# Windowed attention and two MLPs on one core: the order of query tiles, the position of the value products and the step where the MLP begins

## The chip, the cores and the metric

The kernel runs on one core of a Trainium2 chip. The metric is the device time of one execution in microseconds (us); less is better. TensorE is written PE in the rows, VectorE DVE, ScalarE ACT, GpSimd POOL, and SyncE, which issues most of the DMAs, SP.

## The reference

```python
B, H, Sl, D = 4, 8, 512, 64;  Sg = 32;  window = 32
# attention: 32 global and 512 local positions of each of 32 heads
s_g  = scale * q_g @ concat(k_g, k_l).T            # global queries see all 544 keys
out_g = softmax(s_g) @ concat(v_g, v_l)
s_ll = where(|i - j| <= window, scale * q_l @ k_l.T, -1e9)
s_lg = scale * q_l @ k_g.T                         # local queries see the 32 global keys
out_l = softmax(concat(s_lg, s_ll)) @ concat(v_g, v_l)
x = concat(out_g, out_l) as [B, 544, 512]
# first MLP, 512 -> 2048 -> 512, with layer norm and residual
x = x + relu(((x - mu) / sqrt(var + 1e-6) * g_ln) @ w_ch1) @ w_ch2
# second MLP, 512 -> 1024 -> 512, with a 3-tap convolution over positions as a gate
h = relu(x @ w_in);  out = (h * sigmoid(conv3(h))) @ w_out
```

All inputs and the output are float32.

## The kernel before, in words

Every engine's program is one loop over the same steps `s` (0 to END-1). Each step has slots for several pieces of work, and semaphores order the engines; no scheduler moves anything, so the order written in the loop is the order on the engine.

**Attention** takes steps 0 to 66. Step s treats two heads (a pair p of heads, kept together in `two[...]` and `vv[...]`) and one tile t of 128 local queries. On TensorE a step holds `scores(s)` (2 matmuls with 64 rows of contraction; they stand in the trace as tiles 64\*128), `transposes(s-2)` (4 transposes of the exponentials, 128\*128) and `values(s-3)` (16 small matmuls into 32-partition pieces of the output bank, 128\*32). Between them DVE takes the masked row maximum (`row_max`, L736), ACT the exponentials (`exponents`, L926 and L929) and the copy of the transposed exponentials out of PSUM (`probabilities`, L952). After each second step DVE divides by the row sums (`read_out`, L768 to L776) into `x_loc`. For each group G of four heads there are also the global queries: `global_scores` (8 matmuls, called a burst here), `global_max`, `global_exponents`, two extra transposes (G0, G1) and `global_values`. From G = 2 on the scores of the burst's step come late in it, behind the MLP's up-projection.

**The MLP** has 104 units: `up(n)` (12 matmuls of 256 or 384 columns, from the layer-normed x and the hi and lo parts of the weights) and `down(n)` (6 or more matmuls of 512 columns). Unit n stands in step `U0 + n`, and `down` one step later. With U0 = 23, steps 23 to 66 hold attention and MLP together. PSUM is short: before U0 attention alternates between two banks for transposes and for outputs, and the same banks are `u_ps` for the MLP from U0 on, after which each has one bank. Row statistics (`half_sums`, `variances` on DVE, `inverse_deviation` on POOL), `ln_rows` on DVE, and the transposes called LN come for all four tiles of a batch at once. Weights are split in `scale_up` (DVE), `weights_hi` (ACT, L986) and `weights_lo` (POOL, L1078), at the steps of `W_STEP`.

What sets the start of the MLP is written in two places: the layer-normed tiles must be there, and the PSUM bank must have been read.

```python
if n < N1 and f == 0:
    pe.wait_ge(tlo_ok, LOWS[max(T_IDX[("LN", t)] for t in tiles)])
```

Of the kernel before, what the change touches and what calls it, by code (L numbers as in the profile page):

```python
# [10 lines left out]
P = 128  # L11
# [17 lines left out]
SLOTS, PSLOTS, HSLOTS = 4, 4, 3  # L29

U0 = 23
# [15 lines left out]

def ln_step(t):  # L50
    return 75 if t == GT else 16 * (t // QT + 1) + 5 + t % QT
# [12 lines left out]
def extras(s):  # L64

    found = []
    if s % 8 == 1 and 0 <= (s - 9) // 8 < NGROUPS:
        found.append(("G0", (s - 9) // 8))
    if s % 8 == 2 and 0 <= (s - 10) // 8 < NGROUPS:
        found.append(("G1", (s - 10) // 8))  # L70
    if s in LN_AT:
        found.append(("LN", LN_AT[s]))
    if s in Y_AT:
        found.append(("Y", Y_AT[s]))
    return found


def global_values_in(s):
    return (s - 11) // 8 if s % 8 == 3 and 0 <= (s - 11) // 8 < NGROUPS else None


def burst_in(s):
    return s // 8 - 1 if s % 8 == 0 and 0 <= s // 8 - 1 < NGROUPS else None
# [18 lines left out]
def score_bank(s):  # L102

    return int(s < U0 and s % 2 == 1 and s not in (9, 17))

# [23 lines left out]
def o_head(m):  # L129
    return m + m // GH  # L130


def o_group(G):
    return 5 * G + 4


O_FLIP = 10
# [24 lines left out]
def stats_before(b):  # L162
    return 13 * b
# [3 lines left out]
W_STEP = ([5, 7, 9, 13, 15, 17, 21, 23] + [70 + 2 * j for j in range(8)]  # L167
# [8 lines left out]
def attention_mlp(nc, kq2, vx, wall, gln, convw, ident, maskp, outT):  # L176
# [9 lines left out]
    with ctx:  # L186
# [10 lines left out]
        minus_half = sb(ctx, "minus_half", [P, QT])  # L197
        bst = sb(ctx, "bst", [P, QT, 2, 6])
        mv = sb(ctx, "mv", [P, QT, 2])
        bn_gate = sb(ctx, "bn_gate", [P, 1])  # L200
        veps = sb(ctx, "veps", [P, QT])
        rstd = sb(ctx, "rstd", [P, QT])
# [96 lines left out]
        stat_ok, rstd_ok, lnn_ok = sem("stat_ok"), sem("rstd_ok"), sem("lnn_ok")  # L299
        xn_out = [sem(f"xn_out{r}") for r in range(2)]  # L300
# [47 lines left out]
        def _(sp):  # L348
            def load_two(p):
                if p >= SLOTS:  # L350
                    sp.wait_ge(gs_ok, (p - SLOTS) // 2 + 1)
                sp.dma_start(two[p % SLOTS][:, :], kq2[p]).then_inc(kq_in[p % SLOTS], 16)

            def load_v(p):
                if p >= SLOTS:
                    sp.wait_ge(pv_ok, V_IDX[("G", (p - SLOTS) // 2)] + 1)
# [3 lines left out]
            def v_load_step(p):  # L360
                return 4 * p - 6 if p < SLOTS else 8 * ((p - SLOTS) // 2) + 12
# [21 lines left out]
            def load_xg():  # L383
                sp.wait_ge(pv_ok, len(V_SEQ))
# [82 lines left out]
            load_two(1)  # L467
            load_v(1)
            sp.dma_start(g_sb[:, :], gln).then_inc(const_in, 16)
            sp.dma_start(conv_sb[:, :, :], convw).then_inc(const_in, 16)  # L470
            for s in range(END):
                for p in range(2, TWOS):
                    if 4 * p - 8 == s:
                        load_two(p)
                    if v_load_step(p) == s:
                        load_v(p)
                for j in range(24):
                    if w_load_step(j) == s:
                        load_w(j)
                if s % 8 == 4 and 0 <= (s - 12) // 8 < NGROUPS:  # L480
                    store_global((s - 12) // 8)
# [3 lines left out]
                if s == 68:  # L485
# [4 lines left out]
                for e in range(TILES):  # L490
                    c = min(e // 2, 7)
                    if s == U0 + HALF * (c + 1) + 2:
                        store_y1(e)
                for k in range(1, len(CH2)):
                    if s == (0, 77, 90, 104, 112)[k]:
# [15 lines left out]
        def _(pe):  # L511
# [3 lines left out]
            def scores(s):  # L515
                p, t = divmod(s, QT)
# [4 lines left out]
                if s % 8 == 0 and s // 8 - 1 >= 2:  # L521
                    pe.wait_ge(gexp_ok, s // 8)
                if s in (11, 19):
                    pe.wait_ge(gexp_ok, s // 8)
# [6 lines left out]
            def global_scores(G):  # L531
                pe.wait_ge(bias_ok, 16 * (G + 1))
# [43 lines left out]
            def values(gp):  # L576
                p, t = divmod(gp, QT)
# [118 lines left out]
            for s in range(END):  # L696
# [22 lines left out]
                if 0 <= s - 3 < PAIRS:  # L719
                    values(s - 3)  # L720
# [6 lines left out]
        def _(dve):  # L727
# [3 lines left out]
            def row_max(s):  # L731
# [3 lines left out]
                for j in range(2):  # L735
                    v.tensor_tensor_reduce(m_sb[s % 2][:, 256 * j:256 * (j + 1)], s_bank(s, j),  # L736
                                           maskb[:, (s % QT + 1) // 2, :],
# [23 lines left out]
            def read_out(m):  # L761

                k, r, u = o_head(m), m % 2, m % 2
                b, p = divmod(m // 2, HEADS // 2)
# [26 lines left out]
            def half_sums(b, half):  # L791
                dve.wait_ge(o_ok, o_head(HEADS * b + GH * half + 3) + 1)
                if half == 0 and b > 0:
                    dve.wait_ge(lnn_ok, QT * b)
                for t in range(QT):
                    v.bn_stats(bst[:, t, half, :], x_loc[b % 2][:, t, 256 * half:256 * (half + 1)]).then_inc(stat_ok, 1)

            def global_sums():
                dve.wait_ge(xg_in, 16)
                dve.wait_ge(lnn_ok, QT * BATCH)  # L800
                v.bn_stats(bst[:, 0, 0, :], x_g[:, :]).then_inc(stat_ok, 1)

            def variances(b):
                n, halves = (1, 1) if b == BATCH else (QT, 2)
                dve.wait_ge(stat_ok, stats_before(b) + n * halves)
                v.memset(bn_gate[:, :], 0.0)
                for t in range(n):
                    v.bn_aggr(mv[:, t, :], bst[:, t, 0:halves, :].rearrange("p a b -> p (a b)")).then_inc(stat_ok, 1)
                dve.wait_ge(stat_ok, stats_before(b) + n * halves + n)
                v.tensor_scalar_add(veps[:, 0:n], mv[:, 0:n, 1], 1e-6).then_inc(stat_ok, 1)  # L810

            def ln_rows(t):
                b, r = divmod(t, QT)
                i = LN_ORDER.index(t)
                dve.wait_ge(rstd_ok, b + 1)
# [57 lines left out]
            for s in range(END):  # L873
# [6 lines left out]
                for t in range(TILES):  # L880
                    if s == ln_step(t) - 1 - (t == GT) - (t % QT == 1):
                        ln_rows(t)
# [18 lines left out]
                if s % 16 == 11 and s // 16 < BATCH:  # L901
                    half_sums(s // 16, 0)
                if s % 16 == 3 and 1 <= s // 16 <= BATCH:
                    half_sums(s // 16 - 1, 1)
                    variances(s // 16 - 1)
                if s == 72:
                    global_sums()
                    variances(BATCH)
# [8 lines left out]
        def _(act):  # L917
# [122 lines left out]
            for s in range(END):  # L1040
# [29 lines left out]
        def _(pool):  # L1070
# [10 lines left out]
            def inverse_deviation(b):  # L1081
                n = 1 if b == BATCH else QT
                pool.wait_ge(stat_ok, stats_before(b) + (3 if b == BATCH else 13))
                g.tensor_tensor(rstd[:, 0:n], veps[:, 0:n], minus_half[:, 0:n], ALU.pow).then_inc(rstd_ok, 1)
# [11 lines left out]
            for s in range(END):  # L1096
                if s - 1 in W_AT:
                    weights_lo(W_AT[s - 1])
                if s % 16 == 3 and 1 <= s // 16 <= BATCH:
                    inverse_deviation(s // 16 - 1)  # L1100
                if s == 72:
                    inverse_deviation(BATCH)
# [67 lines left out]
```

## Time and profile before

| | |
|---|---|
| median of 3 runs | 762.49 us (761.04 to 763.51) |
| the profiled execution: own time / span in the trace | 762.49 us / 760.7 us |
| TensorE busy (modelled, pipelined) | 746.1 us, 98% |
| VectorE / ScalarE / GpSimd busy | 44% / 39% / 18% |
| DMA | 88.03 MB, mean 116 GB/s |

A matmul's busy time is longer than the distance to the next one's start, since matmuls are pipelined. The price of a piece of work on TensorE is therefore read here from start to start, in rows in order of time. A matmul of float32 on float32 data stands as two records, so that a step's 2 score matmuls are "x4" and its 16 value matmuls "x32".

### The profile page before, as it was taken

Reading aid. Unit: us, or ns where it says so; the run is one execution under the profiler, and the core shown is the slowest. Engines: PE = TensorE matmul, PEld = TensorE weight load, DVE = VectorE, ACT = ScalarE, POOL = GpSimd, SP = SyncE. Lnnn points to the kernel's source line nnn. Section 1 sums busy time; section 2 is a strip of 40 time slices with the busy share of each in tenths; the row PEclk is TensorE's granted clock in tenths of the full one; section 3 lists DMA queues with packets and bytes.
Section 4 is the critical chain, followed back from the end, with each engine's and each line's share of the span. In section 5 each row is a group of like instructions: output and inputs, shape, how many; then the busy total and the mean of one; then the engine's idle time right before and its main releaser. Section 6 shows DMA issues by size and latency. Waiting matters only on the chain.

```text
span 760.7 us, 16627 instructions
## 1 busy us (share of the span) xinstructions
PE 746.1 (98%) x6802; PEld 638.4 (84%) x6802; DVE 336.3 (44%) x901; ACT 295.1 (39%) x758; POOL 139.3 (18%) x114
## 2 busy tenths in 40 slices
PE   8989999999999999999999999999989999999998
PEld 4656777777777778998989998888889999999997
DVE  4766434443354424422122222113167776677764
ACT  6977354453545442432122221111133433433343
POOL 0342000000000000432032430110202232223222
PEclk9999999999999999999999999999999999999999
DMA  9575414242253002362623683522533212221200
GB/s 329 177 275 167 149 49 161 60 121 92 65 177 112 4 29 98 113 193 73 205 68 107 187 262 114 168 82 63 160 116 114 74 46 89 62 88 34 86 31 30
DMA packets 84428, 88.03 MB, mean 116 GB/s; under 512 B 8832, under 2 KB 66432, under 8 KB 84352
## 3 DMA queue, kind: packets, MB, share of 16 engines
q1 hardware_dynamic: 83984, 86.37, 35.4%
q8 instruction: 54, 0.88, 0.5%
q10 hardware_dynamic: 368, 0.59, 0.3%
q14 instruction: 22, 0.18, 0.1%
HBM read 57.33 MB, written 29.62 MB: 114 GB/s over the span
## 4 chain that ended last, share of the span: by engine, by line
PE 94%; ACT 2%; DVE 1%; DMA 1%; issue 1%; POOL 0%; ACTq 0%; DVEq 0%
PE u_ps L513 38%; PE y_ps L513 27%; PE s_ps L513 17%; PE t_ps L554 6%; PE o_ps L513 5%; DMA identf<-in_ident 1%; PE u_ps L554 1%; ACT e_sb L926 1%; ACT probs L952 0%; ACT w_hi L986 0%; ACT e_sb L929 0%; POOL hb L1093 0%; ACT xn L968 0%; ACT y_sb L1033 0%; DVE xn L752 0%
## 5 line engine op out<-in xcount | busy, mean ns | idle before, releaser
L841 DVE SCALAR_TENSOR_TENSOR hb<-u_ps,hb 128x384 fp32r<-128x384 f32 (+1 forms) x48 | 28.9, 602 | 175.9 <-ACT hb L996 175.9
L513 PE MATMUL u_ps<-xc,w_hi 128*128 128x274 f32 x512 | 100.2, 290 | 0.0
L996 ACT ACTIVATE hb<-u_ps 128x384 fp32r<-128x384 f32 (+1 forms) x48 | 25.3, 527 | 175.4 <-PE u_ps L513 175.4
L858 DVE SCALAR_TENSOR_TENSOR conv_h<-relu_h,conv_sb,conv_h 128x272 f32<-128x272 f32 x128 | 88.7, 693 | 4.6
L513 PE MATMUL u_ps<-xn,w_hi 128*128 128x256 f32 x448 | 86.6, 291 | 0.1
L1093 POOL TENSOR_TENSOR hb<-gated,hb 128x272 fp32r<-128x272 f32 x64 | 54.9, 858 | 156.4 <-ACT hb L1026 156.4
L513 PEld LDWEIGHTS u_ps<-xc,w_hi 128*128 128x128 f32 x512 | 81.5, 190 | 0.2
L952 ACT COPY probs<-t_ps 128x512 f32<-128x512 f32 (+1 forms) x67 | 36.5, 546 | 103.5 <-PE t_ps L554 103.3
L1078 POOL TENSOR_TENSOR w_lo<-w_raw,w_hi 128x1024 fp32r<-128x1024 f32 x22 | 52.6, 2390 | 127.9 <-ACT w_hi L986 127.9
L513 PE MATMUL u_ps<-xc,w_lo 128*128 128x274 f32 x256 | 74.5, 291 | 0.0
L1012 ACT ACTIVATE relu_h<-u_ps 128x274 f32<-128x274 f32 x64 | 25.7, 401 | 122.0 <-PE u_ps L513 122.0
L513 PE MATMUL u_ps<-xb,w_hi 128*128 128x384 f32 (+1 forms) x256 | 72.1, 363 | 0.0
L513 PEld LDWEIGHTS u_ps<-xn,w_hi 128*128 128x128 f32 x448 | 69.9, 191 | 2.0 <-DVE xn L752 0.5
L736 DVE CUSTOM_DVE_ANT_0 m_sb<-s_ps,maskb 128x256 f32<-128x256 f32 x110 | 42.2, 421 | 51.9 <-PE s_ps L513 51.9
L513 PE MATMUL u_ps<-xn,w_lo 128*128 128x256 f32 x224 | 63.2, 282 | 0.0
L841 DVE SCALAR_TENSOR_TENSOR h_lo<-u_ps,h_hi 128x256 fp32r<-128x256 f32 x56 | 23.8, 424 | 88.5 <-ACT h_hi L996 88.5
L513 PE MATMUL y_ps<-w_hi,hb 128*128 128x512 f32 x192 | 60.8, 398 | 0.0
L926 ACT ACTIVATE e_sb<-m_sb,nbias 128x128 f32<-128x128 f32 x128 | 51.0, 398 | 11.6 <-DVE nbias L736 11.6
L513 PEld LDWEIGHTS u_ps<-xb,w_hi 128*128 128x128 f32 x256 | 47.6, 188 | 6.3
L513 PE MATMUL y_ps<-hb,w_hi 128*128 128x272 f32 x256 | 51.6, 292 | 0.7 <-POOL hb L1093 0.7
L513 PE MATMUL s_ps<-hb,w_hi 128*128 128x272 f32 x256 | 50.6, 288 | 0.0
L929 ACT ACTIVATE e_sb<-m_sb,nbias 128x128 f32<-128x128 f32 x128 | 50.2, 392 | 0.0
(109 smaller groups left out, 1505.8 us busy)
## 6 DMA issues: line engine op xcount, KB each, us to landing
w_raw<-in_wall SPq DMA_DIRECT2D x22, 512.0 KB, 3.8
two<-in_kq SPq DMA_DIRECT2D x15, 640.0 KB, 5.9
xc<-y_parts SPq DMA_DIRECT2D x8, 1092.0 KB, 5.8
vv<-in_vx SPq DMA_DIRECT2D x16, 520.0 KB, 6.5
y_parts<-yT SPq DMA_DIRECT2D x16, 512.0 KB, 3.5
xn_parts<-xn SPq DMA_DIRECT2D x14, 512.0 KB, 3.4
xb<-xn_parts SPq DMA_DIRECT2D x14, 512.0 KB, 6.6
y_first<-y_sb SPq DMA_DIRECT2D x17, 256.0 KB, 4.8
```

Of the source, the lines that this page charges most:

```text
L513: return nc.tensor.matmul(out, lhsT, rhs, start=start, stop=stop)
L554: last = nc.tensor.transpose(t_ps[T_BANK[k]][:, P * c:P * (c + 1)], src, identf[:, :])
L736: v.tensor_tensor_reduce(m_sb[s % 2][:, 256 * j:256 * (j + 1)], s_bank(s, j), maskb[:, (s % QT + 1) // 2, :], -D ** -0.5, -MASKED, ALU.add ...
L841: v.scalar_tensor_tensor(out=lo, in0=u_ps[n % 2][:, 0:width], scalar=0.0, in1=hi.bitcast(f32), op0=ALU.max, op1=ALU.subtract).then_inc(hlo ...
L858: v.scalar_tensor_tensor(out=cv, in0=h[:, n:CN + n], scalar=conv_sb[:, f, n:n + 1], in1=cv, op0=ALU.mult, op1=ALU.add).then_inc(cv_ok, 1)
L926: nc.scalar.activation(e[:, P:].rearrange("p (a b) -> p a b", b=64), m[:, 64:192].rearrange("p (a b) -> p a b", b=64), ACT.Exp, bias=nbias ...
L929: last = nc.scalar.activation(e[:, 0:P].rearrange("p (a b) -> p a b", b=64), m.rearrange("p (a b) -> p a b", b=64)[:, 0:4:3, :], ACT.Exp, ...
L952: nc.scalar.copy(probs[slot][:, 0:width], t_ps[T_BANK[k]][:, 0:width]).then_inc(thi_ok, 1)
L996: nc.scalar.activation(h_parts(n)[0], u_ps[n % 2][:, 0:width], ACT.Relu).then_inc(hhi_ok, 1)
L1012: nc.scalar.activation(relu_h[sc % 4][:, :], u_ps[sc % 2][:, 0:CW], ACT.Relu).then_inc(relu_ok, 1)
L1078: g.tensor_tensor(w_lo[at][:, :], w_raw[W_SLOT[j]][:, :], w_hi[at][:, :].bitcast(f32), ALU.subtract).then_inc(wlo_ok, 1)
L1093: g.tensor_tensor(hb[sc % HSLOTS][:, 1, 0:CN], gated[sc % 2][:, :], hb[sc % HSLOTS][:, 0, 0:CN].bitcast(f32), ALU.subtract).then_inc(clo_o ...
```

## The change

- Queries: with `place(s)` two query tiles of all four head pairs of a batch come first (8 steps), then the other two tiles. Each key/query load is used for 2 steps, and again 8 steps later, so `two` and `vv` get eight slots, and `probs` five.
- Norm: statistics and layer norm are done for two tiles, every 8 steps, and the MLP's unit 0 moves from step 23 to 15 (`U0`), with the weight steps, loads and stores that hang on it.
- On TensorE, `values(s-3)` and `global_values` stand directly behind `scores(s)`, ahead of `transposes(s-2)`; before, `values` stood behind the up-projection.
- The burst of group G moves from step 8G+8 to 8G+2, its extra transposes and values to 8G+4, 8G+5 and 8G+7. ACT does a step's exponentials before the burst's.

```diff
-SLOTS, PSLOTS, HSLOTS = 4, 4, 3
+SLOTS, PSLOTS, HSLOTS = 8, 5, 3
-U0 = 23
+U0 = 15
+def place(s):
+    b, r = divmod(s, 16)
+    u, r = divmod(r, 8)
+    return 4 * b + r // 2, 2 * u + r % 2
+GT_STEP = 68
 def ln_step(t):
-    return 75 if t == GT else 16 * (t // QT + 1) + 5 + t % QT
+    return GT_STEP if t == GT else 8 * (t // 2) + 13 + t % 2
 def burst_in(s):
-    return s // 8 - 1 if s % 8 == 0 and 0 <= s // 8 - 1 < NGROUPS else None
+    return s // 8 if s % 8 == 2 and s // 8 < NGROUPS else None
 def o_head(m):
-    return m + m // GH
+    return m + (m + 2) // GH
-O_FLIP = 10
+O_FLIP = 6
-W_STEP = ([5, 7, 9, 13, 15, 17, 21, 23] + [70 + 2 * j for j in range(8)]
+W_STEP = ([7, 9, 11, 13, 15, 16, 17, 19] + [67 + 2 * j for j in range(8)]
...
                 if G is not None:
                     global_scores(G)
+                if global_values_in(s) is not None:
+                    global_values(global_values_in(s))
+                if 0 <= s - 3 < PAIRS:
+                    values(s - 3)
                 if 0 <= s - 2 < PAIRS:
                     transposes(s - 2)
-                if global_values_in(s) is not None:
-                    global_values(global_values_in(s))
...
                 if s < PAIRS and late:
                     scores(s)
-                if 0 <= s - 3 < PAIRS:
-                    values(s - 3)
...
-            def half_sums(b, half):
-                dve.wait_ge(o_ok, o_head(HEADS * b + GH * half + 3) + 1)
+            def half_sums(c, half):
+                dve.wait_ge(o_ok, o_head(4 * c + 2 * half + 1) + 1)
...
+                if s < PAIRS and not late:
+                    exponents(s)
                 if G is not None:
                     global_exponents(G)
-                if s < PAIRS and not late:
-                    exponents(s)
```

On TensorE in a step with attention and MLP together, before. The names are: `y_ps` the down-projection, `s_ps` scores, `t_ps` transposes, `u1_ps` and `u0_ps` the up-projection, `o_ps` value products.

```order
L513 MATMUL y_ps<-w_lo6,h_hi0 128x512
L513 MATMUL s_ps<-two3 128x256 x2
L554 MATMUL t_ps<-identf,e_sb1 128x128 x4
L513 MATMUL u0_ps<-xn1,w_hi0 128x256 x2
...
L513 MATMUL u0_ps<-xn1,w_lo0 128x256
L513 MATMUL o_ps<-vv3,probs2 32x65 x16
L513 MATMUL y_ps<-w_hi7,h_hi1 128x512
```

The same engine and kind of step, of the change:

```order
L529 MATMUL y_ps<-w_lo0,h_hi2 128x512
L529 MATMUL s_ps<-two4 128x256 x2
L529 MATMUL o_ps<-vv7,probs3 32x65 x16
L572 MATMUL t_ps<-identf,e_sb1 128x128 x4
L529 MATMUL u0_ps<-xn1,w_hi2 128x256 x2
...
L529 MATMUL u0_ps<-xn1,w_lo2 128x256
L529 MATMUL y_ps<-w_hi1,h_hi0 128x512
```

The value products moved from between up and down to between scores and transposes.

On TensorE at the program's start (steps 2 to 4), before; here `u1_ps` and `t_ps` are the two banks of the transposes:

```order
L513 MATMUL s_ps<-two0 128x256 x2
L513 MATMUL u0_ps<-probs3 128x512 x3
L554 MATMUL t_ps<-identf,e_sb0 128x128 x4
L513 MATMUL y_ps<-two0 128x256 x2
L554 MATMUL u1_ps<-identf,e_sb1 128x128 x4
L513 MATMUL o_ps<-vv0,probs0 32x65 x16
L513 MATMUL s_ps<-two1 128x256 x2
```

And of the change:

```order
L529 MATMUL s_ps<-two1 128x256 x2
L529 MATMUL u0_ps<-probs4 128x512 x3
L529 MATMUL y_ps<-two0 32x320 x2
L529 MATMUL y_ps<-two1 32x320 x2
L529 MATMUL y_ps<-two0 32x320 x2
L529 MATMUL y_ps<-two1 32x320 x2
L572 MATMUL t_ps<-identf,e_sb0 128x128 x4
L529 MATMUL s_ps<-two1 128x256 x2
L529 MATMUL o_ps<-vv0,probs0 32x65 x16
L572 MATMUL u1_ps<-identf,e_sb1 128x128 x4
```

The first burst (`32x320`) now stands ahead of the first transposes, and the scores of step 2 need the second pair of heads (`two1`), not the first.

## Rows read from the trace of the kernel before

**Rows 1.** Stretches: busy us of PE, PEld, DVE, ACT, POOL; then TensorE's granted clock.

```profile
9.00:37.00 28.00, 26.33 (x554) 17.37 (x556) 18.62 (x81) 26.36 (x74) 7.08 (x3) 1.00 0.68 252
47.00:61.00 14.00, 12.37 (x225) 8.28 (x228) 9.19 (x40) 9.24 (x26) 3.45 (x3) 0.76 0.69 241
```

**Rows 2.** PE in order of time, a step of attention alone: start us, us, what.

```profile
33.19 0.70 PE L513 MATMUL y_ps<-two 64*128 64x256 f32 x4
33.83 0.66 PE L554 MATMUL u_ps<-identf,e_sb 128*128 128x128 f32 x4
34.41 0.66 PE L513 MATMUL o_ps<-vv,probs 128*32 128x65 f32 x32
35.00 0.49 PE L513 MATMUL s_ps<-two 64*128 64x256 f32 x2
```

**Rows 3.** ACT in order of time in the same stretch.

```profile
33.48 0.40 ACT L926 ACTIVATE e_sb<-m_sb,nbias 128x128 f32<-128x128 f32 x1 [0.18 <-DVE nbias L736]
...
34.66 0.56 ACT L952 COPY probs<-u_ps 128x512 f32<-128x512 f32 x1
```

**Rows 4.** ACT's groups from 9 to 64 us: count, busy us and mean ns.

```profile
L986 ACT CAST w_hi<-w_raw 128x1024 fp32r<-128x1024 f32 x5 | 5.2, 1037 | 0.0
...
L942 ACT ACTIVATE eg_sb<-y_ps,gbias 128x512 f32<-128x512 f32 x2 | 1.4, 680 | 0.0
```

**Rows 5.** PE in order of time: step 2, `up(0)`, the burst of group 3.

```profile
9.10 0.70 PE L513 MATMUL s_ps<-two 64*128 64x256 f32 x4 [0.79 <-DMA identf<-in_ident]
...
63.68 0.49 PE L513 MATMUL u_ps<-xn,w_hi 128*128 128x256 f32 x2
...
108.17 1.28 PE L513 MATMUL s_ps<-two 64*32 64x320 f32 x16
```

**Rows 6.** DMA issues from 2.2 to 2.7 us: KB, us from issue to landing.

```profile
two<-in_kq SPq DMA_DIRECT2D x1, 640.0 KB, 7.3
```

**Rows 7.** PE in order of time, a step with attention and MLP.

```profile
88.78 0.70 PE L513 MATMUL s_ps<-two 64*128 64x256 f32 x4
89.41 0.66 PE L554 MATMUL t_ps<-identf,e_sb 128*128 128x128 f32 x4
89.83 0.48 PE L513 MATMUL u_ps<-xn,w_hi 128*128 128x256 f32 x2
...
91.43 0.66 PE L513 MATMUL o_ps<-vv,probs 128*32 128x65 f32 x32
92.03 0.50 PE L513 MATMUL y_ps<-w_hi,h_hi 128*128 128x512 f32 x1
...
93.63 0.70 PE L513 MATMUL s_ps<-two 64*128 64x256 f32 x4
```

**Rows 8.** PE in order of time, MLP alone: one up-projection, then down.

```profile
320.06 0.40 PE L513 MATMUL u_ps<-xn,w_hi 128*128 128x256 f32 x2
...
321.49 0.40 PE L513 MATMUL y_ps<-w_hi,h_hi 128*128 128x512 f32 x1
```

**Rows 9.** PE in order of time, value products directly behind scores.

```profile
69.98 0.70 PE L513 MATMUL s_ps<-two 64*128 64x256 f32 x4
70.61 0.66 PE L513 MATMUL o_ps<-vv,probs 128*32 128x65 f32 x32
```

**Rows 10.** PE in order of time, a step with global value products (x40).

```profile
84.25 0.79 PE L513 MATMUL o_ps<-vv,probs 128*32 128x65 f32 x40
84.96 0.50 PE L513 MATMUL u_ps<-xn,w_hi 128*128 128x256 f32 x2
```

**Rows 11.** ACT and DVE in order of time in the step of rows 7.

```profile
90.11 0.59 ACT L952 COPY probs<-t_ps 128x512 f32<-128x512 f32 x1 [3.03 <-PE t_ps L554]
...
92.17 0.42 DVE L841 SCALAR_TENSOR_TENSOR h_lo<-u_ps,h_hi 128x256 fp32r<-128x256 f32 x1 [1.86 <-ACT h_hi L996]
...
92.91 0.42 DVE L776 TENSOR_TENSOR x_loc<-o_ps,rsum 128x256 f32<-128x256 f32 x1
```

**Rows 12.** DVE in order of time: lower half of a layer-normed tile (L752).

```profile
62.46 0.69 DVE L752 TENSOR_TENSOR xn<-t_ps,xn 128x512 fp32r<-128x512 f32 x1 [1.07 <-ACT xn L968]
```

More of the change, by code:

```diff
@@ L66, in extras @@
     found = []
[L67 to L70, printed above, removed]
+    if s % 8 == 4 and s // 8 < NGROUPS:
+        found.append(("G0", s // 8))
+    if s % 8 == 5 and s // 8 < NGROUPS:
+        found.append(("G1", s // 8))
     if s in LN_AT:
@@ L102, in score_bank @@
 def score_bank(s):
-    return int(s < U0 and s % 2 == 1 and s not in (9, 17))
+    return int(s < U0 and s % 2 == 1 and s not in (3, 11))
 def score_before(s):
@@ L467, in _ @@
             load_two(1)
+            load_two(2)
             load_v(1)
+            load_two(3)
+            load_v(2)
             sp.dma_start(g_sb[:, :], gln).then_inc(const_in, 16)
@@ L471, in _ @@
             for s in range(END):
-                for p in range(2, TWOS):
-                    if 4 * p - 8 == s:
+                for p in range(4, TWOS):
+                    if first_use(p) - 10 == s:
                         load_two(p)
-                    if v_load_step(p) == s:
+                for p in range(3, TWOS):
+                    if max(first_use(p) - 9, 0) == s:
                         load_v(p)
+                for e in range(TILES):
+                    c = min(e // 2, 7)
+                    if s == U0 + HALF * (c + 1) + 2:
+                        store_y1(e)
                 for j in range(24):
@@ L479, in _ @@
                         load_w(j)
-                if s % 8 == 4 and 0 <= (s - 12) // 8 < NGROUPS:
-                    store_global((s - 12) // 8)
+                if s % 8 == 0 and 0 < s // 8 <= NGROUPS:
+                    store_global(s // 8 - 1)
                 for b in range(BATCH):
@@ L489, in _ @@
                         store_xn(t)
[L490 to L493, printed above, removed]
                 for k in range(1, len(CH2)):
-                    if s == (0, 77, 90, 104, 112)[k]:
+                    if s == U0 + (0, 54, 67, 81, 89)[k]:
                         load_xb(k)
@@ L515, in scores @@
             def scores(s):
-                p, t = divmod(s, QT)
+                p, t = place(s)
                 if t == 0:
@@ L520, in scores @@
                     pe.wait_ge(bias_ok, 2 * (score_before(s) + 1))
[L521 to L524, printed above, removed]
+                if burst_in(s) is not None and burst_in(s) >= 2:
+                    pe.wait_ge(gexp_ok, burst_in(s) + 1)
+                if s in (5, 13):
+                    pe.wait_ge(gexp_ok, s // 8 + 1)
                 for j in range(2):
@@ L803, in variances @@
-            def variances(b):
-                n, halves = (1, 1) if b == BATCH else (QT, 2)
-                dve.wait_ge(stat_ok, stats_before(b) + n * halves)
+            def half_sums(c, half):
+                dve.wait_ge(o_ok, o_head(4 * c + 2 * half + 1) + 1)
+                for t in (2 * c, 2 * c + 1):
+                    v.bn_stats(bst[:, t % QT, half, :],
+                               x_loc[c // 2 % 2][:, t % QT, 256 * half:256 * (half + 1)]).then_inc(stat_ok, 1)
+            def variances(c):
+                at = 2 * (c % 2)
+                dve.wait_ge(stat_ok, stats_before(c) + 4)
+                v.memset(bn_gate[:, :], 0.0)
+                for t in (at, at + 1):
+                    v.bn_aggr(mv[:, t, :], bst[:, t, 0:2, :].rearrange("p a b -> p (a b)")).then_inc(stat_ok, 1)
+                dve.wait_ge(stat_ok, stats_before(c) + 6)
+                v.tensor_scalar_add(veps[:, at:at + 2], mv[:, at:at + 2, 1], 1e-6).then_inc(stat_ok, 1)
@@ L806, in variances, with global_variances @@
+            def global_variances():
+                dve.wait_ge(xg_in, 16)
+                v.bn_stats(bst[:, QT, 0, :], x_g[:, :]).then_inc(gstat_ok, 1)
+                dve.wait_ge(gstat_ok, 1)
                 v.memset(bn_gate[:, :], 0.0)
[L807 to L810, printed above, removed]
+                v.bn_aggr(mv[:, QT, :], bst[:, QT, 0, :]).then_inc(gstat_ok, 1)
+                dve.wait_ge(gstat_ok, 2)
+                v.tensor_scalar_add(veps[:, QT:QT + 1], mv[:, QT:QT + 1, 1], 1e-6).then_inc(gstat_ok, 1)
@@ L880, in _ @@
                 for t in range(TILES):
-                    if s == ln_step(t) - 1 - (t == GT) - (t % QT == 1):
+                    if s == ln_step(t) - 1 - (t != GT and t % 2):
                         ln_rows(t)
@@ L900, in _ @@
                     read_out((s - 4) // 2)
[L901 to L908, printed above, removed]
+                if s % 8 == 7 and s // 8 < 2 * BATCH:
+                    half_sums(s // 8, 0)
+                if s % 8 == 3 and 1 <= s // 8 <= 2 * BATCH:
+                    half_sums(s // 8 - 1, 1)
+                    variances(s // 8 - 1)
+                if s == GT_STEP - 2:
+                    global_variances()
                 if s in W_AT and W_AT[s] < 2 * HALF:
@@ L1079, in weights_lo, with inverse_deviation, global_inverse_deviation @@
                                 ALU.subtract).then_inc(wlo_ok, 1)
[L1081 to L1084, printed above, removed]
+            def inverse_deviation(c):
+                at = 2 * (c % 2)
+                pool.wait_ge(stat_ok, stats_before(c + 1))
+                if c >= 2:
+                    pool.wait_ge(lnn_ok, 2 * (c - 1))
+                g.tensor_tensor(rstd[:, at:at + 2], veps[:, at:at + 2], minus_half[:, at:at + 2],
+                                ALU.pow).then_inc(rstd_ok, 1)
+            def global_inverse_deviation():
+                pool.wait_ge(gstat_ok, 3)
+                g.tensor_tensor(rstd[:, QT:QT + 1], veps[:, QT:QT + 1], minus_half[:, QT:QT + 1],
+                                ALU.pow).then_inc(grstd_ok, 1)
             def residual(q):
@@ L1098, in _ @@
                     weights_lo(W_AT[s - 1])
[L1099 to L1102, printed above, removed]
+                if s % 8 == 3 and 1 <= s // 8 <= 2 * BATCH:
+                    inverse_deviation(s // 8 - 1)
+                if s == GT_STEP - 2:
+                    global_inverse_deviation()
                 if 0 <= s - 2 - C0 < CUNITS:
```

58 lines of the change are left out of this document (29 added, 29 removed).

## Prediction

> **What bounds the kernel now.** The page has TensorE busy for 98% of the span, but that is modelled; start-to-start distances in the order of time tell more. I read the stretches first, then TensorE's rows at either side of step 23, then ACT's and DVE's there.
>
> Steps 0 to 22 hold attention alone. Up to 37 us ACT is busy for 26.36 of 28 us and TensorE for 26.33 [rows 1]: both are near full. A TensorE step costs 0.64 (scores) + 0.58 (transposes) + 0.59 (values) = 1.81 us [rows 2]; ACT's costs 1.18 for the exponentials plus some 0.5 for the copy, 1.7 us [rows 3], and a split weight block adds a cast of 1.04 and a burst 0.68 and more [rows 4]. So ACT's extras overrun the step. From 47 to 61 us TensorE is busy for 12.37 of 14 us and its clock is granted at 0.76 on average, against 1.00 earlier [rows 1]: part of that stretch ran at the lower level (1.2 GHz); it cost 0.24 x 14 = 3.4 us at most. `up(0)` starts at 63.68 [rows 5].
>
> What would TensorE need to get there unhindered? From step 2 at 9.10 [rows 5]: 21 steps of 1.81 (38.0), two bursts of 1.2 (2.4), their extra transposes and values (2.6), two LN transposes (1.1), and 1.0 for scores and transposes of step 23: 54.2. So 9.5 us of the stretch are waits and slow clock. Behind `up(0)` there is little to wait for: a joint step takes 93.63 - 88.78 = 4.85 us, and its pieces follow each other without a gap (0.63 scores, 0.42 transposes, 1.60 up, 0.60 values, 1.60 down) [rows 7].
>
> The joint step holds a second loss. The same up takes 1.43 us when down follows it [rows 8], 1.60 when values follow [rows 7]. Transposes take 0.42 before up [rows 7], 0.58 before values [rows 2]. Entering the 128\*32 value products from a 128\*128 matmul costs about 0.17 us. Behind scores it doesn't show: scores then take 0.63 [rows 9], as they do before transposes.
>
> **The change, part by part.**
>
> 1. *`up(0)` comes earlier.* I walk ACT's copies of the exponentials, one per step, since in the new order they chain: copy(k), then values(k), then transposes(k+1), then copy(k+1). Before, the transposes didn't stand behind the values of the step before. From a transpose's start to the copy's start 0.70, copy 0.59 [rows 11], values 0.59 [rows 2]: 1.9 us a step, 0.1 over today's 1.81. Start: step 2's scores now need the second pair's keys, whose load takes 7.3 us to land [rows 6] and is issued inside the 2.2 to 2.7 window, so about 9.6 instead of 9.10; scores, three warming matmuls (some 0.7), and the first burst of 1.28 [rows 5] ahead of the first transposes: these start at 12.2, the copy at 12.9. Then, copy to copy: steps 3, 6, 9, 11 at 1.9 (7.6); step 2 with the burst's exponentials 2.4; steps 4, 5, 7 with group work 2.2, 2.0, 2.4; step 8 with a cast (its 1.04 overlaps a little) 2.6; step 10 with cast and burst 3.3; step 12 with cast and group copy 3.1; step 13 with group and LN copies 2.5. Sum 28.1, so copy of step 14 at 41.0. Behind it exponentials and copy (1.7), the LN copy (0.55), its lower half on DVE (0.69, [rows 12]), and behind that on DVE the read-out (0.8: from 92.51, where the lower part ends, to 93.33, [rows 11]), for which the global values now wait, since the output bank is single from there: 44.8. Two lots of values and transposes (1.6): **`up(0)` at 46.4 us.** This has 6.2 us of waits in it, against an unhindered 40.2. Bounds: none of them, 40.2; all 9.5 of today's, 49.7. I take 46.4.
>
> 2. *Clock.* Today's two drops follow waits. The longest wait here is again in front of `up(0)`, some 2 us. Bounds: nothing, or today's 3.4 us. I take half, 1.7: `up(0)` acts as if at 48.1. That is **-15.6 us**.
>
> 3. *Work that moves behind `up(0)`.* Eight steps of attention less one lot of values. A joint step in the new order costs 4.85 - 0.17 = 4.68, of which MLP alone is 1.43 [rows 8] + 1.4 (six matmuls of down, 1.60 less the entry to scores): 1.85 for attention, no less than the 1.81 it costs alone. 8 x 1.85 - 0.6 = **+14.2 us**. So putting MLP beside attention is worth nothing by itself; the gain is only in fewer waits.
>
> 4. *Values behind scores.* In the joint steps that exist already (23 to 63, 41 of them, less 5 with a late burst whose values stood behind scores already) 0.17 to 0.18 each: 36 x 0.18 = 6.5. In the six steps with global values, today these stand behind transposes (which then take 0.58), take 0.71 [rows 10] and leave again to up: one more entry and one more exit, 0.33 each, 2.0. In the late bursts scores wait for the exponentials behind up; values ahead of it cover that, 0.5. Sum **-9.0 us**. Bounds: 0 (if the entry is only moved, below) and 9.6.
>
> 5. *New waits in joint steps.* ACT's copy now comes 0.6 later in the step, as transposes do, and high h, low h and read-out with it. Today the read-out ends at 92.91 + 0.42 = 93.33, 4.55 after the step's scores [rows 7, 11]; in the new order 5.15. Values of the next step would start at 4.68 + 0.63 = 5.31. That leaves 0.15 us. In the six even steps with an LN tile the lower half (0.69, [rows 12]) comes ahead of it and some 0.2 is lost each: **+1.0 us**. Bounds: 0, or 0.5 in each of 25 odd steps, 12.
>
> 6. *Slots, loads, norm by two.* Eight slots lift the waits of loads; and DVE's and ACT's in-order programs don't stand behind a load in the joint steps, which last 4.85 us each. Statistics of two tiles instead of four shorten DVE's step 19 (now 11); that is in the walk above. The weights of units 3 to 7 are split in steps 14 to 20 and wanted at 18 to 22; with joint steps of 4.7 us the 1.04 cast [rows 4] and the rest fit. Cost nothing; if POOL were two steps late, some 5 us once.
>
> Sum: -15.6 + 14.2 - 9.0 + 1.0 = **-9.4**. On the profiled execution's 762.49 us, which is also the median: **753.0 us**.
>
> The Trainium skill's page "TensorEngine Tiling (Array Packing)", section Key Properties, says that changing the tiling mode drains TensorE. Scores are 64\*128 and values 128\*32, so by that rule scores to values would be a change too, and the new order would still have three a step for today's four. Read more strictly, that each entry into values costs its 0.17 whatever stands ahead, item 4 would be nothing and the time about 762; the trace disagrees for scores [rows 9].
>
> **Rivals.**
>
> - *The entry cost stays.* If values still cost 0.17 behind scores in steady steps, item 4 falls by 8.5 and item 3 rises by 1.4: 762 to 763. Against it: in rows 9 the scores take 0.63 to the values' start, the same as to transposes in rows 2. Few places show it. Chance 0.04.
> - *The start eats it.* The new copy-values-transposes chain, the early burst and late keys cost 4 us more than I walked, or the clock falls for longer: 756 to 760. For it: TensorE idles a larger part of each step in steps 8 to 14. Chance 0.19.
> - *The start runs well.* No drop of the clock and half the waits: 746.5 to 750. Chance 0.12.
> - *Slower.* The single output bank: values in every odd joint step now come 2.2 us sooner behind the read-out, which stays behind up, high h and low h. The margin is 0.15 us. A read-out 0.53 us later than walked costs 25 waits of 0.38, the whole gain; at 0.7 later it is 25 x 0.55 = 13.8, and the time 767. Against it: all lags are read from a regular step. Chance 0.05.
> - My forecast, 750 to 756: 0.60.
>
> **Numbers.** Within 0.3% (760.2 to 764.8) is about what a measurement of this kernel can't tell from no change. Faster: 0.60 + 0.19 + 0.12 = 0.91, less a little for 756 to 760 running over: 0.89. Same 0.06, slower 0.05. Range 748 to 758.5.
>
> **What the next profile would show.** Right: `up(0)` at 45 to 49 us; joint steps of 4.67 us with up at 1.43; steps of attention alone at 1.9; global steps shortest in the sum; first transposes at 12.2. Wrong: values in odd joint steps released by DVE's `x_loc`; up still 1.6; TensorE's clock low behind `up(0)`; waits for `w_lo` in steps 18 to 22.

## Result, and the profile after

The changed kernel takes 770.91 us (median of 4, 770.56 to 771.18) against 761.8 us for the kernel before on the same chip: a ratio of 1.0116, 95% interval 1.0096 to 1.0136. It is some 9 us slower, where 9.4 us faster was forecast.

The page of the profiled execution of the changed kernel (its own time 770.56 us), first lines and the chain by engine:

```profile
span 768.7 us, 16644 instructions
...
PE 740.1 (96%) x6802; PEld 636.7 (83%) x6802; DVE 337.8 (44%) x909; ACT 295.4 (38%) x758; POOL 140.7 (18%) x118
...
PE 87%; ACT 5%; DVE 3%; issue 3%; DMA 1%; POOL 0%; SPq 0%; ACTq 0%; DVEq 0%
```

No engine has more to do. TensorE's share of the chain that ended last is 87%, where it was 94% before: the share of ACT and DVE in that chain grew from 3% to 8%, so the time went into waits on them. Cut at `up(0)`, the span is 50.9 + 717.8 us, against 63.7 + 697.0 before. So the MLP did start 12.8 us earlier, and what follows it took 20.8 us longer, for a forecast of 6.2.

A regular joint step of the changed kernel, TensorE in order of time:

```profile
96.95 0.70 PE L529 MATMUL s_ps<-two 64*128 64x256 f32 x4
97.58 0.66 PE L529 MATMUL o_ps<-vv,probs 128*32 128x65 f32 x32
98.18 0.66 PE L572 MATMUL t_ps<-identf,e_sb 128*128 128x128 f32 x4
98.59 0.48 PE L529 MATMUL u_ps<-xn,w_hi 128*128 128x256 f32 x2
...
100.10 0.40 PE L529 MATMUL y_ps<-w_hi,h_hi 128*128 128x512 f32 x1
...
101.58 0.49 PE L529 MATMUL s_ps<-two 64*128 64x256 f32 x2
```

101.58 - 96.95 = 4.63 us, where [rows 7] have 4.85: this part came as forecast (4.68), even a little better. It came in two places: up takes 1.51 us here (98.59 to 100.10) for 1.60, and down 1.48 (100.10 to 101.58) for 1.60 behind the values [rows 7]. The loss is in two other steps of each eight. The step with global values, TensorE and then DVE in the same stretch:

```profile
90.46 0.70 PE L529 MATMUL s_ps<-two 64*128 64x256 f32 x4
91.33 0.79 PE L529 MATMUL o_ps<-vv,probs 128*32 128x65 f32 x40 [0.17 <-DVE x_loc L794]
92.96 0.66 PE L529 MATMUL o_ps<-vv,probs 128*32 128x65 f32 x32 [0.84 <-issue]
```

```profile
90.85 0.42 DVE L794 TENSOR_TENSOR x_loc<-o_ps,rsum 128x256 f32<-128x256 f32 x1
...
92.18 0.16 DVE L801 TENSOR_SCALAR rgsum<-o_ps 128x1 f32<-128x1 f32 x1 [0.20 <-PE o_ps L529]
92.38 0.16 DVE L803 RECIPROCAL rgsum<-rgsum 128x1 f32<-128x1 f32 x1
92.58 0.28 DVE L807 TENSOR_SCALAR x_glo<-o_ps,rgsum 128x64 f32<-128x64 f32 x1
```

The ordinary values (x32) start at 92.96, 0.10 us after DVE has finished `x_glo` at 92.86. Both kinds write the one output bank, so the second waits until the first has been read. The row puts the 0.84 us down to "issue"; the two times together show what it is, and eight steps later the same row names the read-out:

```profile
135.94 0.66 PE L529 MATMUL o_ps<-vv,probs 128*32 128x65 f32 x32 [0.89 <-DVE x_glo L807]
```

Together the two kinds take 2.22 us here (91.33 to 93.55). In step 7 of the same kernel, where each has a bank of its own, they take 1.17:

```profile
22.38 0.78 PE L529 MATMUL o_ps<-vv,probs 128*32 128x65 f32 x40
22.99 0.63 PE L529 MATMUL u_ps<-vv,probs 128*32 128x65 f32 x32
23.55 0.66 PE L572 MATMUL u_ps<-identf,e_sb 128*128 128x128 f32 x4
```

So the wait costs 1.05 us. Before, `up` stood between the two [rows 10] and covered the read-out. The global values themselves wait 0.24 us more: scores to values takes 0.87 (90.46 to 91.33) for 0.63.

The second is the step with the last transposes of a group and a layer-normed tile. All engines, in order of time:

```profile
82.35 0.27 PE L572 MATMUL t_ps<-identf,eg_sb 128*128 128x128 f32 x1
...
82.78 0.36 ACT L1020 ACTIVATE h_hi<-u_ps 128x256 fp32r<-128x256 f32 x1
83.04 0.26 ACT L976 COPY probs<-t_ps 128x128 f32<-128x128 f32 x1
...
83.44 0.63 PE L572 MATMUL t_ps<-identf,ln_n 128*128 128x128 f32 x4 [0.82 <-ACT probs L976]
```

The LN transposes need the one transposes bank, which ACT empties only behind the exponentials and `h_hi`: 1.09 us from one transposition to the other. Before, these two stood in different steps (8G+10 for the group, 16b+21 to 16b+24 for LN). Both waits come in each of the six groups of eight joint steps. All that TensorE's matmuls wait for from 50 to 330 us (total us, times, longest):

```profile
PE t_ps L572 <- ACT probs L976: 5.0, 6, 0.8
PE o_ps L529 <- DVE x_glo L807: 2.7, 3, 0.9
PE o_ps L529 <- issue: 2.5, 3, 0.9
PE o_ps L529 <- DVE x_loc L794: 1.6, 8, 0.4
```

The start, in the changed kernel. TensorE in step 15:

```profile
46.96 1.28 PE L529 MATMUL o_ps<-vv,probs 128*32 128x65 f32 x40 [2.26 <-DVE x_loc L794]
49.12 1.10 PE L529 MATMUL o_ps<-vv,probs 128*32 128x65 f32 x32 [0.87 <-DVE x_glo L807]
50.15 1.12 PE L572 MATMUL t_ps<-identf,e_sb 128*128 128x128 f32 x4
50.91 0.56 PE L529 MATMUL u_ps<-xn,w_hi 128*128 128x256 f32 x1
```

And stretches (busy us of PE, PEld, DVE, ACT, POOL, then the granted clock):

```profile
37.00:51.00 14.00, 8.94 (x170) 6.29 (x168) 6.98 (x26) 8.22 (x21) 5.46 (x4) 0.86 0.69 227
47.00:54.00 7.00, 6.13 (x90) 5.52 (x92) 1.20 (x7) 1.90 (x6) 1.82 (x1) 0.51 0.57 157
```

TensorE is busy for 8.94 of the 14 us ahead of `up(0)`, and from 47 to 54 us its granted clock is 0.51, the lower of its two levels (1.2 GHz).

### The profile page after: what moved, and what is told of

The parts are those of the page before. It is cut to its first block, busy times and chain, and to the rows that moved or that the text cites. A ratio compares the mean times of both kernels' runs of the same rounds, so it can differ in the third digit from the quotient of the medians.

```text
span 768.7 us, 16644 instructions
## 1 busy us (share of the span) xinstructions
PE 740.1 (96%) x6802; PEld 636.7 (83%) x6802; DVE 337.8 (44%) x909; ACT 295.4 (38%) x758; POOL 140.7 (18%) x118
## 4 chain that ended last, share of the span: by engine, by line
PE 87%; ACT 5%; DVE 3%; issue 3%; DMA 1%; POOL 0%; SPq 0%; ACTq 0%; DVEq 0%
PE u_ps L529 35%; PE y_ps L529 24%; PE s_ps L529 16%; PE t_ps L572 6%; PE o_ps L529 5%; ACT e_sb L950 2%; ACT e_sb L953 1%; DMA two<-in_kq 1%; DVE xn L770 1%; ACT xn L992 1%; ACT h_hi L1020 1%; DVE x_loc L794 1%; ACT probs L976 1%; ACT w_hi L1010 0%; DVE rsum L788 0%
## 5 line engine op out<-in xcount | busy, mean ns | idle before, releaser
L976 ACT COPY probs<-t_ps 128x512 f32<-128x512 f32 (+1 forms) x71 | 39.6, 558 | 132.3 <-PE t_ps L572 132.3
L529 PE MATMUL u_ps<-xn,w_lo 128*128 128x256 f32 x224 | 63.7, 285 | 0.0
L529 PEld LDWEIGHTS o_ps<-vv,probs 128*32 128x32 f32 x2176 | 35.0, 111 | 33.3 <-issue 23.8
L754 DVE CUSTOM_DVE_ANT_0 m_sb<-s_ps,maskb 128x256 f32<-128x256 f32 x118 | 45.3, 422 | 26.0 <-PE s_ps L529 25.9
L529 PE MATMUL o_ps<-vv,probs 128*32 128x65 f32 x2176 | 45.6, 226 | 10.5 <-DVE x_loc L794 3.8
L950 ACT ACTIVATE e_sb<-m_sb,nbias 128x128 f32<-128x128 f32 x128 | 50.9, 397 | 11.2 <-DVE nbias L754 11.1
```

Source lines behind the costliest of these rows:

```text
L529: return nc.tensor.matmul(out, lhsT, rhs, start=start, stop=stop)
L950: nc.scalar.activation(e[:, P:].rearrange("p (a b) -> p a b", b=64), m[:, 64:192].rearrange("p (a b) -> p a b", b=64), ACT.Exp, bias=nbias ...
L976: nc.scalar.copy(probs[slot][:, 0:width], t_ps[T_BANK[k]][:, 0:width]).then_inc(thi_ok, 1)
```

## Experiments

Each ratio is against the kernel before, on the same chip. The chips differ a little, so times are compared through the ratio.

| run | median us | ratio (95% interval) | span: to up(0) + rest |
|---|---|---|---|
| before | 761.8 to 762.2 | 1 | 63.7 + 697.0 |
| change | 770.91 | 1.0116 (1.0096 to 1.0136) | 50.9 + 717.8 |
| e1, values apart | 763.86 | 1.0021 (1.0011 to 1.0032) | 48.4 + 713.0 |
| e2, groups earlier | 764.81 | 1.0030 (1.0017 to 1.0042) | 51.3 + 711.8 |
| e3, both | 758.29 | 0.9951 (0.9933 to 0.9968) | 49.1 + 707.4 |
| e6, old order at the start | 768.34 | 1.0098 (1.0067 to 1.0130) | 52.9 + 717.7 |
| e7, all mended | 756.84 | 0.9931 (0.9911 to 0.9950) | 46.5 + 708.6 |
| e9, old order everywhere | 762.90 | 1.0011 (0.9996 to 1.0025) | 47.9 + 713.3 |
| e4, before, values moved from 23 | 758.21 | 0.9950 (0.9936 to 0.9965) | 64.6 + 691.9 |
| e5, the same in all steps | 761.31 | 0.9993 (0.9982 to 1.0004) | 67.8 + 691.8 |
| e8, before, values moved from 25 | 755.97 | 0.9926 (0.9911 to 0.9942) | 61.8 + 691.6 |
| f3, e8 and global values first | 756.44 | 0.9928 (0.9909 to 0.9946) | 63.7 + 690.9 |
| f1, e7 and read-out first | 755.55 | 0.9912 (0.9896 to 0.9928) | 48.4 + 708.8 |
| f4, f1 and first burst later | 754.95 | 0.9909 (0.9893 to 0.9926) | 46.2 + 707.1 |

**The two waits, each taken away alone.** The edit of e1, on TensorE:

```diff
-                if 0 <= s - 3 < PAIRS:
+                behind = s >= U0 and global_values_in(s) is not None
+                if 0 <= s - 3 < PAIRS and not behind:
                     values(s - 3)
                 if 0 <= s - 2 < PAIRS:
                     transposes(s - 2)
...
+                if 0 <= s - 3 < PAIRS and behind:
+                    values(s - 3)
                 if 0 <= s - 1 - U0 < N1 + N2:
                     down(s - 1 - U0)
```

> The changed kernel, with one edit: in the joint steps that hold global value products (s % 8 = 7, from step 15), the ordinary value products go back behind the up-projection; the global ones stay behind the scores. Theory BANK: output has one bank from step 15, so the values directly behind the global ones wait until VectorE has read those out; the trace shows 2.23 us for both where 1.17 is their price (91.33 to 93.55). With up between them, that wait of 1.06 goes in 6 steps, and about 1 us in step 15, less 0.17 to 0.33 for a second entry and exit each: -5 to -6 us, from 770.9 to about 765 to 766. Rival CHAIN: the joint steps are held by the chain over ScalarE and VectorE, and the wait only moves to the transposes or the next scores: 770 to 771.

Measured: 763.86, ratio 1.0021: 7 us under the change, where 5 to 6 were expected. `up(0)` came 2.5 us earlier: 1.5 of that is the 0.87 wait and the values (0.6) gone from ahead of it, the rest is that the clock fell later in this execution (0.76 from 47 to 54 us for 0.51). The global steps behind it take 5.80 us for 6.50, six times 0.7. Some 1 us more was gained in the second MLP, which the edit doesn't touch; no run shows why.

The edit of e2, in `extras`:

```diff
-    if s % 8 == 4 and s // 8 < NGROUPS:
+    if s % 8 == 3 and s // 8 < NGROUPS:
         found.append(("G0", s // 8))
-    if s % 8 == 5 and s // 8 < NGROUPS:
+    if s % 8 == 4 and s // 8 < NGROUPS:
         found.append(("G1", s // 8))
```

> The changed kernel, with the two extra transposes of a group one step earlier (s % 8 = 3 and 4 for 4 and 5), so that none stands in a step with an LN transpose. Theory BANK: the LN transposes wait for ScalarE's copy of the group's small transpose, since transposes have one bank in joint steps; 1.10 us from one to the other where 0.20 is the price (82.35 to 83.44). That is 0.9 in 6 joint steps: -5 to -5.5 us, about 765.5; and some more before step 15, where ScalarE had both in step 13. Rival CHAIN: ScalarE gets its work earlier but the wait comes back at another transposition: 770 to 771.

Measured: 764.81, ratio 1.0030: 6 us under the change, a little more than the 5 to 5.5 expected. `up(0)` is at 51.3, so all of it came behind that; the further gain that was expected ahead of it didn't show. Run e3 has both edits.

> The changed kernel with both edits that paid alone: values apart from global values in joint steps (-7.0 us alone), and the group's extra transposes one step earlier (-6.1 alone). Theory BANK: the two waits are separate, so the gains add: 770.9 - 13 = 758, faster than the kernel before. Rival: with one wait gone the other resource (ScalarE and VectorE in turn) holds the step, and the sum is under 9: 762 or more.

Measured: 758.29, ratio 0.9951. The gains add within the noise: 13.2 us by the medians of the two singly, 12.6 together, and behind `up(0)` 4.8 and 6.0 singly, 10.4 together. So theory BANK holds and the rival, a chain that would bring the waits back elsewhere (under 9 us), falls. TensorE in e3's step with global values:

```profile
87.68 0.70 PE L529 MATMUL s_ps<-two 64*128 64x256 f32 x4
88.55 0.79 PE L529 MATMUL o_ps<-vv,probs 128*32 128x65 f32 x40 [0.16 <-DVE x_loc L797]
89.27 0.66 PE L572 MATMUL t_ps<-identf,e_sb 128*128 128x128 f32 x4
...
91.28 0.66 PE L529 MATMUL o_ps<-vv,probs 128*32 128x65 f32 x32
91.88 0.50 PE L529 MATMUL y_ps<-w_hi,h_hi 128*128 128x512 f32 x1
```

The global values take their 0.72 us now, and the ordinary ones start without a wait. The 0.87 from scores to global values for 0.63 is the one wait that was forecast (0.2 us).

**The value products alone, in the kernel before.** The same move, with U0 still 23, one query tile at a time as before, and the steps with a late burst or global values left alone:

```diff
+                first = s >= U0 and not late and global_values_in(s) is None
+                if 0 <= s - 3 < PAIRS and first:
+                    values(s - 3)
                 if 0 <= s - 2 < PAIRS:
                     transposes(s - 2)
...
-                if 0 <= s - 3 < PAIRS:
+                if 0 <= s - 3 < PAIRS and not first:
                     values(s - 3)
```

> The kernel before, with one part of the change alone: in joint steps (from 23), other than those with a late burst or global values, the value products go directly behind the scores. 35 steps. If the switch into the value products' tiling is what I read (about 0.2 us a step, seen as 4.63 for 4.85 us in the changed kernel's regular steps), the time falls by 7 to 7.7 us, from 761.8 to about 754.3, with nothing lost anywhere. Rival: the read-out of the single output bank comes too late for values that start 2.2 us earlier, and the gain is under 4 us.

Measured: 758.21, ratio 0.9950: 3.8 us faster, half of what was expected, and just inside the rival's "under 4". The rest behind `up(0)` fell by 5.1 us: regular steps take 4.62 to 4.67 us for 4.85, and the read-out that the rival had in mind holds only one joint step in sixteen, for 0.28 us (scores to values 0.91, at 144.80). `up(0)` itself came 0.9 later, at 64.6. TensorE in e4's step 23:

```profile
59.81 0.70 PE L513 MATMUL s_ps<-two 64*128 64x256 f32 x4
62.82 1.10 PE L513 MATMUL o_ps<-vv,probs 128*32 128x65 f32 x32 [2.30 <-issue]
63.84 1.12 PE L554 MATMUL t_ps<-identf,e_sb 128*128 128x128 f32 x4
64.61 0.78 PE L513 MATMUL u_ps<-xn,w_hi 128*128 128x256 f32 x2
```

The values wait 2.3 us ahead of the transposes and `up(0)`. Before, they stood behind both. `up(0)` then ran at the lower clock, 2.11 us for 1.52, which is part of the rest. Run e8 begins the new order with step 25 (`first = s > U0 + 1 and ...`).

> The kernel before with values behind scores in joint steps, but from step 25 on, not in steps 23 and 24. In the run from 23 on, the first up-projection came at 64.6 us instead of 63.7, since in step 23 the values, now ahead of it, waited 2.4 us for a read-out. Account: 1 us of that comes back, 757.2 or less. Rival: the start has nothing to do with it, 758.2.

Measured: 755.97, ratio 0.9926, 5.6 us faster than before and 2.2 under e4, where 1 us or more was expected. TensorE in e8's step 23:

```profile
59.14 0.70 PE L513 MATMUL s_ps<-two 64*128 64x256 f32 x4
61.45 0.63 PE L554 MATMUL t_ps<-identf,e_sb 128*128 128x128 f32 x4 [1.61 <-DVE xn L755]
61.84 0.48 PE L513 MATMUL u_ps<-xn,w_hi 128*128 128x256 f32 x2
```

From scores to `up(0)` 2.70 us pass, for 4.80 in e4. The rest is e4's (691.6 for 691.9), so the two differ ahead of `up(0)` alone. Run e5 moves them in the steps of attention alone as well (`first` without `s >= U0`).

> As the run before it, but also in the steps of attention alone (0 to 22, without the step with global values). My prediction's chain, copy to values to transposes to the next copy, says 1.9 us for a step instead of 1.81, so the part before the first up-projection takes 1 to 3 us more: about 756. Rival: ScalarE is the bound there anyway, and the time is that of the run before, 754.3.

Measured: 761.31, ratio 0.9993: all of e4's gain but 0.5 us is gone, and it went ahead of `up(0)` (67.8 for 64.6; the rest is equal). TensorE in e5's steps of attention alone:

```profile
14.62 0.70 PE L513 MATMUL y_ps<-two 64*128 64x256 f32 x4
15.37 0.66 PE L513 MATMUL u_ps<-vv,probs 128*32 128x65 f32 x32
15.96 0.65 PE L554 MATMUL u_ps<-identf,e_sb 128*128 128x128 f32 x4
16.54 0.70 PE L513 MATMUL s_ps<-two 64*128 64x256 f32 x4
```

16.54 - 14.62 = 1.92 us a step for 1.81 [rows 2]. It fits the chain from copy to values to the next transposes, which the prediction put at 1.9. From step 3 to step 21 e5 loses 1.9 us on e4, and 1.7 more from there to `up(0)`, where TensorE waits longer and its clock fell earlier (0.91 for 1.00 from 47 to 61 us).

**The start of the changed kernel.** Run e6 gives the changed kernel the old order in steps 0 to 14 (`behind = s < U0`).

> The changed kernel, in steps 0 to 14 (attention alone) with the old order of scores, transposes, values. The run with values behind scores in those steps of the kernel before was 3.1 us slower than the one without (761.3 to 758.2). Theory CHAIN-START: there the copy of the exponentials, the values and the next transposes stand in one chain, 1.9 us or more a step, so the first up-projection comes 1 to 3 us earlier here: 768 to 769.5. Rival: what holds the start is the early burst and ScalarE, and nothing moves: 771.

Measured: 768.34, ratio 1.0098, with an interval that holds the change's 1.0116. The direction is as expected, the size (1.4 us) isn't settled. Its profiled execution was the longest of the four (772.45) and had more stretches at the lower clock (0.94 from 9 to 37 us for 1.00), so its `up(0)` at 52.9 says little. A better pair is e3 and e7 below, which up to step 14 differ in nothing else: the scores of step 15 start at 44.16 and 43.78 us. So the old order at the start is worth 0.4 us at most, and less than the 1 to 3 us expected.

**MLP from step 15 without the new order.** Run e9: the change with e2's edit, and values behind up, global values behind transposes, in all steps.

> The changed kernel with the group's transposes one step earlier and the old order of TensorE in all steps (scores, transposes, up, values, down), so that what is left of the change is two tiles first, norm by two tiles and MLP from step 15. My account: up(0) some 16 us earlier, eight joint steps more at 2.0 us of attention each (+15.5), no other gain: 761 to 763, no change against the kernel before. Rival: beginning the MLP earlier does pay, 757 or less; or costs, 766 or more.

Measured: 762.90, ratio 1.0011 (0.9996 to 1.0025): no change against the kernel before. 15.8 us come off ahead of `up(0)` and 16.3 are added behind it. Up to unit 60, when attention is over, it is 17.6, 1.05 of that in `up(0)` itself, at the lower clock (2.65 us for 1.60); the second MLP, which has the same instructions, then took 1.2 less than in the kernel before, as in e1. Attention takes about as much of TensorE beside the MLP as alone.

**Mended versions.** Run e7 puts together e1, e2 and e6, and in step 15 both lots of values behind up:

```diff
+                g_at, v_at = (1, 2) if s < U0 else (2, 2) if s == U0 else (0, 2 if gv is not None else 0)
```

(0: behind scores, 1: behind transposes, 2: behind up; first for the global, then for the ordinary values.)

> The changed kernel with the group's transposes one step earlier, values apart from global values in joint steps, the old order in steps 0 to 14, and in step 15 both lots of values behind the up-projection, so that the first up-projection doesn't wait for the read-out. By adding: 758 for the first two, -1.5 for the start, -2 for step 15: 754.5, 7 us faster than the kernel before. If the waits come back elsewhere: 758 or more.

Measured: 756.84, ratio 0.9931; `up(0)` at 46.5. That is 1.5 us under e3 and 2.3 over what was expected: of the 3.5 us hoped for from the start, 2.6 show ahead of `up(0)`, and the rest behind it is 1.2 longer than e3's, since the global values and the wait behind them now stand there too. Three more, on this and on e8. The edit of f3 (on e8): in global steps from 25 on, global values directly behind scores and ordinary ones behind up. Of f1 (on e7), on DVE: `read_out` ahead of `extra_low` where s % 8 = 6. Of f4 (on f1): `transposes` ahead of the first `global_scores`.

> As the run before it, and in the joint steps with global values these go directly behind scores, with the ordinary values behind up, where the read-out of the single bank is covered: one switch less in 6 steps, 0.2 us each: 1.2 us under the run before it, 756. If the read-out before it isn't done in time, nothing or a loss.

> The mended version of the change, with VectorE's read-out ahead of the lower half of the LN tile in the steps s % 8 = 6. Global values then don't wait in the next step: scores to values 0.55 becomes 0.31 (86.54 to 87.09) in 6 steps: -1.4 us, from 756.8 to 755.4. Rival: the LN tile's lower half, 0.8 us later, holds the next transposes, and the sum is nothing.

> As the run before it, and in step 2 the first transposes ahead of the first burst. ScalarE then gets its first copy at about 11.8 instead of 13.1 us. If ScalarE is the bound of the start, up(0) comes 1 us earlier: 754.4. Rival: the later group work takes it back, 755.4.

Measured: f3 0.9928, e8's time; f1 0.9912 and f4 0.9909, both inside e7's interval and each other's. The times alone settle none of the three expectations. The traces show more. f4's step with global values:

```profile
85.91 0.70 PE L529 MATMUL s_ps<-two 64*128 64x256 f32 x4
86.54 0.79 PE L529 MATMUL o_ps<-vv,probs 128*32 128x65 f32 x40
87.26 0.66 PE L572 MATMUL t_ps<-identf,e_sb 128*128 128x128 f32 x4
```

In f1 and f4 scores to global values takes 0.63 us for e7's 0.87, and the step 5.56 for 5.80. So f1's edit does what was expected, and f4's rest is 1.5 us under e7's at the same clock. f3's global steps take 5.56 us for e8's 5.76, as expected too, in five of the six. f4's own edit brings the first transposes 1.3 us forward, but `up(0)` only 0.3: its rival holds. f4, 754.95 us, is the fastest, and 1 us from e8, which changes nothing of the kernel before but the place of the value products: the intervals don't separate them.

What blurs the times is the clock. e8 and f3 have the same instructions up to step 26. TensorE's granted clock from 47 to 61 us, first in e8, then in f3:

```profile
47.00:61.00 14.00, 10.20 (x238) 6.80 (x227) 9.86 (x41) 10.52 (x29) 3.41 (x2) 1.00 0.83 277
```

```profile
47.00:61.00 14.00, 12.29 (x217) 8.19 (x220) 9.16 (x40) 9.22 (x25) 3.43 (x3) 0.76 0.70 240
```

In e8 `up(0)` starts at 61.84 (its row stands above), and in f3:

```profile
63.69 0.48 PE L513 MATMUL u_ps<-xn,w_hi 128*128 128x256 f32 x2
```

The same program gets there 1.85 us earlier; 0.37 of that is there already at step 2 (8.73 and 9.10 us), and the rest came with the clock. e7 and f1 show it more cleanly. They have the same instructions up to step 21 and step 2 at 9.81 and 9.82 us, and `up(0)` is at 46.47 with the clock at 1.00 from 9 to 47 us, and at 48.35 with 0.94 from 9 to 37 and 0.92 from 37 to 47.

## Why the prediction was wrong

By its own steps:

1. *`up(0)` earlier.* Forecast 46.4 at full clock, with 1.7 us for the clock. The changed kernel has 50.9. The walk had the first transposes at 12.2 (they are at 12.38) and the global values of step 15 at 44.8; they start at 46.96. 1.7 of these 2.2 us were lost by the copy of step 14, at 42.7 for 41.0: 0.5 between the copies of steps 9 and 10 (2.4 for 1.9; the burst stands between them), 0.7 between those of 13 and 14 (3.2 for 2.5), the rest in small parts. Then it left out a wait: in step 15 the ordinary values wait for the global ones' read-out (0.87 in the rows above). The rest is work at the lower clock. e7, with the old order at the start, the group's transposes earlier, no values ahead of `up(0)` and no fall of the clock, has 46.5; that this is the forecast's number is luck, since its path is another.
2. *Clock.* Forecast half of today's 3.4 us; 47 to 54 us ran at 0.51, which is 3.4 us at most, since waits stand in it. 1.4 of it fell into `up(0)` itself and the scores behind it.
3. *Work moved behind `up(0)`: +14.2.* Right in kind: with the old order's dearer step (2.0 instead of 1.85) this account gives 15.6, and e9 has 16.6 up to unit 60 without what its `up(0)` lost to the clock. There is no change in the sum.
4. *Values behind scores: -9.0.* The term for a regular step was near, with some luck. It was read from up in the MLP alone (1.43) against up in a joint step (1.60). But up behind transposes and ahead of down takes 1.51, so entering the values from it costs 0.09 and not 0.17; what the prediction left out is down, which takes 0.12 longer behind values than behind up. Together they are the 0.22 of a regular step, for 0.17 to 0.18. In the kernel before, the same move took 5.1 us off behind `up(0)` (e4), 5.7 without what `up(0)` lost to the clock, for 6.5. The 0.5 for late bursts didn't come: up to late scores still takes 1.78 us. The 2.0 for the six steps with global values is there, but hidden: such a step takes 6.50 us, and without its two waits (1.05 and 0.24) it would take 5.21, for 5.75 before.
5. *New waits in joint steps: +1.0.* **This is the step that failed.** It followed each unit through the single output bank for the ordinary read-outs only, and the single transposes bank not at all. What was there: the ordinary values wait for the global read-out, 1.05 us, and the LN transposes for the copy of the group's last ones, 0.89 (1.09 for 0.20). Each comes six times, some 11.6 us together. e1 and e2 took them away one by one for 7 and 6 us (e1 with 2.5 at the start), and both together for 12.6. The wait that was forecast, 0.2 in the even steps with an LN tile, was 0.24, seen in the global step behind them; f1 took it away.
6. *Slots, loads, norm by two: nothing.* Right: in the list of waits from 50 to 330 us stands none for the weights' split and none for a load.

With 5 as measured and the start as it was, the sum is -12.8 + 14.2 - 8.5 (4 without the late bursts) + 11.6 + 1.4 (six times 0.24) + 1.4 (`up(0)` at the lower clock, in the rest) = +7.3, against 8.0 between the two spans. What is left is not placed; it is less than the 1 us that e9 takes over the account of 3.

The rivals looked at the right bank but at the wrong neighbour: the "slower" one had the read-out of ordinary values late in every odd step, and the regular steps show no such wait. The one on the drain at scores to values falls too: 0.63 from scores to values, the step at 4.63.

## What to carry to other kernels

When a piece of work moves on an in-order engine, list each resource that it shares (here two PSUM banks that become single at a given step) and, for each step of the pattern, who uses it directly before and after it in the new order; what stood between them until now was the cover of a read-out by another engine. A periodic schedule has to be checked in each of its phases, since the regular one can gain while two out of eight lose more. And where two changes come in one, price them apart: here the position of the value products is worth some 5 us by itself (5.1 and 5.4 behind `up(0)` in e4 and e8), and the earlier start of the MLP nothing that e9 shows: what it takes off ahead of `up(0)` it adds behind.

## What the runs showed of the hardware

- In a regular joint step, entering the 128\*32 value products from up costs 0.09 us (up 1.60 for 1.51), entering them from transposes 0.16 to 0.17 (0.58 for 0.42), and down takes 0.12 longer behind them (1.60 for 1.48). Scores, at 64\*128, take 0.63 ahead of them as ahead of transposes. The Trainium skill, "TensorEngine Tiling (Array Packing)", Key Properties, has each change of the tiling mode drain TensorE. The trace agrees in so far as the new order has three changes in a step for four and takes 0.22 us less. Out of scores both orders change the mode, so the rows show only that the two changes take the same time, and not what one costs.
- Two executions of the same instructions differ by 1.88 us in the first 48 us (e7 and f1, 46.47 and 48.35), one with TensorE's granted clock at 1.00 throughout and the other with stretches at 0.92 and 0.94.
